# Attention ahead of two mixture-of-experts layers: block averages of the values with the values as the stationary operand

## Chip, cores and metric

The kernel runs on one core of one Trainium2 chip. The metric is the device time of one launch in microseconds. The kernel before took 1074.11 us, the median of three timed runs (1064.62, 1074.11 and 1075.32 us).

## What is computed

Inputs are q, k and v of shape (4, 8, 768, 64), 4 batch elements with 8 heads, float32, and the weights of two expert layers. The change is in the attention alone:

```python
block, window = (32, 16)
nb = S // block                                   # 24 blocks of 32 keys
k_sum = k.reshape(B, H, nb, block, D).max(axis=3)
v_sum = v.reshape(B, H, nb, block, D).mean(axis=3)
scores_l = scale * np.matmul(q, k.transpose(0, 1, 3, 2))       # masked to |i - j| < 16
scores_s = scale * np.einsum('bhsd,bhnd->bhsn', q, k_sum) + np.log(block)
a = softmax(np.concatenate([masked scores_l, scores_s], axis=-1))
out = np.matmul(a, np.concatenate([v, v_sum], axis=2))
```

Each query attends to the keys nearer than 16 and to 24 block summaries: the maximum of each block's keys, the mean of each block's values. Its output, 3072 tokens of 512, goes through a layer of 8 experts (each token to its best expert, hidden size 1024) and a second such layer in which each expert takes 384 tokens.

## The kernel before

One program, with an instruction stream written out by hand for each of five engines (TensorE, VectorE, ScalarE, GpSimd, called POOL in the profile, and SyncE, called SP), tied by semaphores. The stages follow each other: attention, routing of the first layer, its experts, routing of the second layer and its experts interleaved.

**Work of the attention.** The heads are taken in pairs (hp, four pairs for each of four batch elements, 16 pairs in all). A pair has 12 query blocks of 64 (j); a block sees a span of 96 keys (`WK`) and the 24 block summaries, 120 rows (`PW`) in all. The values come from the host cut into these spans, `va[hp]`: 96 rows of keys, then 24 rows in which the block means are put. For each query block and head they hold 64 values and a column of ones, which gives the softmax's denominator in the same matmul.

A pair is three units (n = 3 hp, 3 hp + 1, 3 hp + 2) of four query blocks. The units are software-pipelined with one order on every engine, in the functions `unit` of each block. In unit n TensorE issues: `scores(n)` (L670), `transpose_probs(n-2)` (L679), then, if n % 3 is 1, `means` of the next pair m (L689), then `values(n-3)` (L707), `transpose_rows(n-4)` (L721) and, for each batch element's last pair, the router's `first_logits(n-5)` (L730). VectorE: `maxima(n)` (L1231, L1234), `take_means` (L1204) if n % 3 is 1, `normalise(n-3)` (L1240, L1242, L1247), and `block_maxima` (L1186) of the next pair's keys. ScalarE does the exponentials and the copies out of PSUM. POOL works by pairs: `key_spans(m)` (L518, L519, L521) cuts the keys into spans, `spread_means(m)` (L528) spreads the means over the 12 blocks of `va`. The loop over the first three batch elements is a hardware loop; the first 6 units stand before it and the last element's behind it.

**The means before.** `average` is a table of 96 x 12 x 24 numbers made on POOL (L534, four times L532): 1/32 where a span's key row belongs to a block. For each of the 12 spans a matmul has the 24 columns of `average[:, j, :]` stationary (weights) and 128 columns of values (two heads) moving, and all 12 add up in 24 rows (96 to 119) of a PSUM bank, `MEAN0` onwards, in the bank that `values(n-3)` of the same unit writes. `take_means` copies them to `vst`, waiting for that unit's values (`pv_done`), and `spread_means` copies `vst` into `va`. `values` of the pair wait for that (`vsum_done`).

In float32 each such matmul is two passes on TensorE: the profile counts two MATMUL (PE) and two LDWEIGHTS (PEld) for one; its transposes are one pass.

Of the kernel before, what the change touches and what calls it, by code (L numbers as in the profile page):

```python
# [10 lines left out]
ALU = mybir.AluOpType  # L11
# [4 lines left out]
P = 128  # L16
B, H, S, D = 4, 8, 768, 64
BLOCK, WINDOW = 32, 16
NB = S // BLOCK
# [20 lines left out]
MEAN0 = 2 * GU * VD  # L40
MASKED = -1e30
# [71 lines left out]
def two_layers_of_experts(nc, queries, k, v_win, modality_id, w_gate, modality_bias, w1, w2,  # L113
                          w_gate2, w1b, w2b, out):
    ctx = ExitStack()
    with ctx:
# [133 lines left out]
        means_made = sem("means_made")  # L250
        means_taken = sem("means_taken")
# [38 lines left out]
        average = sa("average", [WK, NQ, NB])  # L290
# [4 lines left out]
        va = [sa(f"va{i}", [PW, 2, NQ, VD]) for i in range(HP)]  # L295
# [106 lines left out]
        def _(sp):  # L402
# [4 lines left out]
            def load_v(b, hp):  # L407
                sp.dma_start(va[hp][0:WK, :, :, :], v_win[bass.ds(b, 1), hp, :, :, :, :].rearrange("o p h j w -> (o p) h j w")
                             ).then_inc(vw_loaded[hp], 16)
# [78 lines left out]
        def _(pool):  # L488
# [35 lines left out]
            def spread_means(m):  # L524
                pool.wait_ge(means_taken, m + 1)
                if m >= HP:
                    pool.wait_ge(pv_done, PU * (m - HP + 1))
                chain(g.tensor_copy(va[m % HP][WK:PW, :, :, 0:D], vst[m % 2][WK:PW, :, :].unsqueeze(2).to_broadcast([NB, 2, NQ, D])))  # L528
                g.nop().then_inc(vsum_done, 1)

            avg = average[:, :, :]
            pick = lambda pattern, base, per: chain(g.affine_select(out=avg, in_=avg, compare_op=ALU.is_ge, fill=0.0, base=base,  # L532
                                                                    pattern=pattern, channel_multiplier=per))
            chain(g.memset(avg, 1.0 / BLOCK))  # L534
            pick([[QB, NQ], [-BLOCK, NB]], -WINDOW, 1)
            pick([[-QB, NQ], [BLOCK, NB]], WINDOW + BLOCK - 1, -1)
            pick([[-2, NQ], [1, NB]], 0, 0)
            pick([[2, NQ], [-1, NB]], 1, 0)
            for t in va:
                chain(g.memset(t[WK:PW, :, :, D:VD], 1.0))  # L540
# [113 lines left out]
        def _(pe):  # L654
# [38 lines left out]
            def values(b, n):  # L693

                hp, i = n // PU, n % PU
                if i == 0:
                    pe.wait_ge(vsum_done, HP * b + hp + 1)
                pe.wait_ge(pt_out, UNITS * b + n + 1)
                if n >= 2:
                    pe.wait_ge(x_done, UNITS * b + n - 1)  # L700
                else:
                    pe.wait_ge(means_taken, 2)
                for t in range(GU):
                    for h in range(2):
                        a = 2 * t + h
                        for s_ in range(2):
                            last = mm(bank[4 + n % 2][QB * s_:QB * s_ + QB, VD * a:VD * a + VD], pt[n % 2][:, a, QB * s_:QB * s_ + QB],  # L707
                                      va[hp % HP][:, h, 2 * (GU * i + t) + s_, :], start=True, stop=True)
                last.then_inc(pv_done, 1)
# [27 lines left out]
            def unit(b, n, own):  # L737
# [4 lines left out]
                if n == 0:  # L742
                    pe.wait_ge(const_ready, 1)
                    means(0, 0, 0)
                if n % PU == 1:
                    m = n // PU + 1
                    own(means, PU * m, m, n)
# [418 lines left out]
        def _(dve):  # L1166
# [30 lines left out]

            def take_means(b, m, n):
# [37 lines left out]
            def normalise(b, m):  # L1236
                hp, i = m // PU, m % PU
                ps = bank[4 + m % 2][:, 0:2 * GU * VD].rearrange("p (a w) -> p a w", w=VD)
                dve.wait_ge(pv_done, UNITS * b + m + 1)
                vec.tensor_scalar(rtmp[:, :], ps[:, :, D], 1e-9, None, ALU.add).then_inc(sums_read, 1)  # L1240
# [3 lines left out]
                if i == 0:  # L1244
# [3 lines left out]
                                  ps[:, :, 0:D].rearrange("p (t h) d -> p t h d", h=2),  # L1248
                                  rinv[:, :].rearrange("p (t h) -> p t h", h=2).unsqueeze(3).to_broadcast([P, GU, 2, D]), ALU.mult).then_inc(x_done, 1)

            def unit(b, n, own):

                own(maxima, n, n)
                m = n // PU + 1
                if n == 0:
                    take_means(0, 0, 0)
                if n % PU == 1:
                    own(take_means, PU * m, m, n)
# [460 lines left out]
def laid_out(inputs):  # L1719
# [9 lines left out]
    rows = _np.ones((B, HP, WK, 2, NQ, VD), v.dtype)  # L1729
    rows[..., :D] = _np.where(outside[:, :, None], 0, v[:, :, :, key, :]).transpose(0, 1, 4, 2, 3, 5)  # L1730
# [26 lines left out]
```

## Time and profile before

| | |
|---|---|
| median of three timed runs | 1074.11 us |
| lowest and highest | 1064.62, 1075.32 us |
| the profiled execution's own time | 1066.68 us |
| its span, first to last instruction | 1064.9 us |
| TensorE busy | 898.2 us, 84% |
| VectorE busy | 681.6 us, 64% |
| mean granted TensorE clock | 0.925 of 2.4 GHz |

The profile is of one execution. PE is TensorE's matmuls, PEld its weight loads, which run beside them; DVE is VectorE, ACT ScalarE. An "L" number is a line of the kernel. "Idle before" is time in which the engine stood still ahead of an instruction, with what ended it. The granted clock is 1.00 at 2.4 GHz and 0.50 at 1.2 GHz. Two levels are all that occur. Times within the span are counted from its first instruction.

### The profile page before, as it was taken

The numbers are of one execution on the slowest core, as the hardware profiler recorded it, in microseconds if no ns is written. First come the engines' busy times: TensorE is split into PE (matmuls) and PEld (weight loads), VectorE is DVE, ScalarE is ACT, GpSimd is POOL, SyncE is SP. The second block draws the span as 40 slices with busy tenths as digits, with TensorE's granted clock in tenths as the row PEclk, the third lists the DMA queues.
The fourth block names the chain that finished last, engine by engine and source line by source line (L and its number), as shares of the span: only waits on it lengthen the run. The fifth ranks groups of instructions, "written<-read, shape, count | busy, mean of one in ns | idle before, by whom it ended". The sixth has DMA issues, their size and how long they took to land.

```text
span 1064.9 us, 21948 instructions
## 1 busy us (share of the span) xinstructions
PE 898.2 (84%) x7342; PEld 733.7 (69%) x7343; DVE 681.6 (64%) x1998; ACT 305.5 (29%) x626; POOL 285.1 (27%) x390
## 2 busy tenths in 40 slices
PE   4899999915899999999996233999898989998995
PEld 3787878714688888888885122868686867687884
DVE  5757576575666666666665567777777768674440
ACT  2544454505322212222221003223232322223330
POOL 5733344101012111111220005050515151414501
PEclk9999999956899999999998655999999999999998
DMA  9676675915011111111110123414141414155100
GB/s 195 122 160 135 133 153 100 280 50 185 11 51 40 50 40 40 40 40 40 40 50 20 24 71 119 159 51 169 50 169 54 165 61 159 61 204 172 32 29 30
DMA packets 45631, 99.94 MB, mean 94 GB/s; under 512 B 6736, under 2 KB 19072, under 8 KB 45440
## 3 DMA queue, kind: packets, MB, share of 16 engines
q1 hardware_dynamic: 26816, 61.63, 19.8%
q0 software_dynamic: 8064, 26.46, 7.9%
q10 hardware_dynamic: 10688, 11.01, 4.9%
q8 instruction: 39, 0.64, 0.2%
q14 instruction: 24, 0.20, 0.1%
HBM read 79.57 MB, written 19.51 MB: 93 GB/s over the span
## 4 chain that ended last, share of the span: by engine, by line
PE 69%; DVE 18%; issue 4%; POOL 3%; ACT 2%; DMA 2%; DVEq 0%; ACTq 0%; SPq 0%; POOLq 0%
PE bank L777 27%; PE bank L898 11%; PE bank L912 9%; PE bank L689 4%; PE bank L670 3%; PE bank L848 3%; DVE w_low L1649 2%; PE bank L730 2%; PE bank L707 2%; PE bank L801 2%; PE bank L679 2%; POOL slot_hot L635 2%; DVE xl L1653 1%; DVE ge L1517 1%; ACT xh L1042 1%
## 5 line engine op out<-in xcount | busy, mean ns | idle before, releaser
L1404 DVE SCALAR_TENSOR_TENSOR bank<-y,wg 128x512 f32<-128x512 f32 x200 | 132.0, 723 | 2.9
L635 POOL TENSOR_SCALAR slot_hot<-iota_l,mlo 128x128 bf16<-128x128 f32 x96 | 72.0, 766 | 214.7 <-DVE mlo L1622 214.7
L898 PE MATMUL bank<-xh,w_high 128*128 128x384 f32 x256 | 94.3, 368 | 16.1 <-DVE hl L1639 8.9
L777 PE MATMUL bank<-w_high,hh 128*128 x200 | 83.2, 416 | 13.2 <-DVE hl L1393 13.2
L777 PE MATMUL bank<-w_high,xh 128*128 x200 | 82.7, 414 | 10.7 <-DVE gates L1386 10.7
L592 POOL DMA_INDIRECT y_rows<-y,sidx x25 | 25.0, 998 | 243.2 <-DVE bank L1404 243.2
L898 PE MATMUL bank<-xh,w_low 128*128 128x384 f32 x256 | 88.1, 344 | 0.0
L898 PE MATMUL bank<-xl,w_high 128*128 128x384 f32 x256 | 87.9, 344 | 0.0
L1042 ACT ACTIVATE hh<-bank 128x512 fp32r<-128x512 f32 x50 | 27.1, 595 | 203.1 <-PE bank L801 203.1
L1418 DVE TENSOR_SCALAR y<-bank,gates 128x512 f32<-128x512 f32 x25 | 18.8, 751 | 101.1 <-PE bank L777 101.1
L912 PE MATMUL bank<-w_high,hh 128*128 128x512 f32 x192 | 82.3, 429 | 0.0
L1042 ACT ACTIVATE w_high<-w_landed 128x1024 fp32r<-128x1024 f32 x64 | 63.1, 1049 | 66.0 <-DMA w_landed<-in_moe_w 66.0
L777 PE MATMUL bank<-w_low,hh 128*128 x200 | 80.5, 403 | 0.0
L777 PE MATMUL bank<-w_high,hl 128*128 x200 | 80.3, 402 | 0.0
L777 PE MATMUL bank<-w_low,xh 128*128 x200 | 80.3, 402 | 0.0
L777 PE MATMUL bank<-w_high,xl 128*128 x200 | 80.2, 401 | 0.0
L1649 DVE TENSOR_TENSOR w_low<-w_landed,w_high 128x1024 fp32r<-128x1024 f32 x64 | 77.8, 1219 | 0.8
L848 PE MATMUL bank<-ge,cb 128*8 128x16 bf16 x1344 | 42.3, 170 | 41.7 <-DVE ge L1517 41.6
L912 PE MATMUL bank<-w_high,hl 128*128 128x512 f32 x192 | 75.7, 394 | 0.0
L912 PE MATMUL bank<-w_low,hh 128*128 128x512 f32 x192 | 75.5, 393 | 0.0
L848 PEld LDWEIGHTS bank<-ge,cb 128*8 128x8 bf16 x1344 | 36.2, 83 | 54.6 <-DVE ge L1517 50.8
L1118 ACT ACTIVATE hh<-bank 128x384 fp32r<-128x384 f32 x64 | 31.5, 492 | 140.2 <-PE bank L898 140.2
(285 smaller groups left out, 1932.5 us busy)
## 6 DMA issues: line engine op xcount, KB each, us to landing
w_landed<-in_moe_w SPq DMA_DIRECT2D x16, 2048.0 KB, 10.5
va<-in_v_win SPq DMA_DIRECT2D x16, 585.0 KB, 6.4
raw_w<-in_moe_w SPq DMA_DIRECT2D x4, 2048.0 KB, 11.3
k_raw<-in_k SPq DMA_DIRECT2D x16, 384.0 KB, 9.1
q_eye<-in_q ACTq DMA_DIRECT2D x16, 384.0 KB, 7.4
x_rows<-x ACTq DMA_DIRECT2D x12, 384.0 KB, 10.2
wg<-in_moe_w_gate SPq DMA_DIRECT2D x1, 2048.0 KB, 25.8
x_rows<-x SPq DMA_DIRECT2D x4, 387.0 KB, 7.2
```

The source lines that it names most:

```text
L592: pool.indirect_dma_start(out=dst[:, :], out_offset=bass.IndirectOffsetOnAxis(ap=sidx[:, 0:1], axis=0), in_=y[:, 0:w], in_offset=None).the ...
L635: last = g.tensor_scalar(slot_hot[:, j, :], iota_l[:, :], mlo[:, j:j + 1], None, ALU.is_equal)
L670: last = mm(bank[n % 2][QB * s_:QB * s_ + QB, PW * (2 * t + h):PW * (2 * t + h) + PW], qe[hp % 2][:, h, QB * j:QB * j + QB], kbt[hp % 2][: ...
L689: last = mm(bank[4 + (n + 1) % 2][WK:PW, MEAN0:MEAN0 + 2 * D], average[:, j, :], va[m % HP][0:WK, :, j, 0:D], start=j == 0, stop=j == NQ - 1)
L777: last = mm(ps, lhs[a][:, c, :], rhs[b](c), start=c == 0 and t == 0, stop=c == n - 1 and t == 2)
L848: last = mm(bank[7][0:E, 0:KSEARCH], cb[:, j, :], ge[:, j, :], start=j == 0, stop=j == TC - 1)
L898: last = mm(bank[fc % 2][:, 0:CAP], w[:, q % 2, c, f], a[:, c, :], start=c == 0 and t == 0, stop=c == KC - 1 and t == 2)
L912: last = mm(bank[2 + t % 2][:, :], a[:, c, rows], w[:, q % 2, c, :], start=c == 0 and n == 0, stop=c == FC - 1 and n == 2)
L1042: copy = lambda o, a: nc.scalar.activation(o, a, ACT.Copy)
L1118: nc.scalar.activation(hh2[:, fc, :], bank[fc % 2][:, 0:CAP], ACT.Relu).then_inc(hhigh_done, 1)
L1404: stt(bank[6 + e % 2][:, :], y[:, 0:DM], 1.0, wg2[:, e, :], ALU.mult, ALU.mult, accum_out=y[:, DM + e:DM + e + 1]).then_inc(l2_out, 1)
L1649: tt(low, whole, high.bitcast(F32), ALU.subtract).then_inc(low_done, 1)
```

## The change

The averaging matmul is turned round. The values of one span, 128 columns (both heads), are now the stationary operand, and `average` is 96 x 2: a span starts 16 keys ahead of its 64 queries, and rows 16 to 47 and 48 to 79 are its two blocks. Each of the 12 matmuls (`block_sums`) gives two columns of 128 (the block means of both heads, head dimension down the partitions); together they fill 24 columns of a bank, 128 x 24. VectorE copies them to `v_sums` (`take_sums`), and one unit later a single matmul against the identity (`means`, stationary `v_sums`, two passes) turns them into the 24 x 128 that there was before. So that the stationary operand is one row of 128 in memory, `va` is laid out anew: for each span a column of ones, 64 values of head 0, 64 of head 1, a column of ones. `normalise` reads its denominators and values at their new places. The host lays out `v_win` to match, with the same number of bytes.

```diff
-        average = sa("average", [WK, NQ, NB])
+        average = sa("average", [WK, 2])
+        vsums = [sa(f"v_sums{i}", [P, NB]) for i in range(2)]
...
-        va = [sa(f"va{i}", [PW, 2, NQ, VD]) for i in range(HP)]
+        va = [sa(f"va{i}", [PW, NQ, 2 * VD]) for i in range(HP)]
...
-                chain(g.tensor_copy(va[m % HP][WK:PW, :, :, 0:D], vst[m % 2][WK:PW, :, :].unsqueeze(2).to_broadcast([NB, 2, NQ, D])))
+                chain(g.tensor_copy(va[m % HP][WK:PW, :, 1:1 + 2 * D], vst[m % 2][WK:PW, :, :].rearrange("p h d -> p (h d)").unsqueeze(1).to_broadcast([NB, NQ, 2 * D])))
...
             chain(g.memset(avg, 1.0 / BLOCK))
-            pick([[QB, NQ], [-BLOCK, NB]], -WINDOW, 1)
-            pick([[-QB, NQ], [BLOCK, NB]], WINDOW + BLOCK - 1, -1)
-            pick([[-2, NQ], [1, NB]], 0, 0)
-            pick([[2, NQ], [-1, NB]], 1, 0)
+            chain(g.affine_select(out=avg, in_=avg, compare_op=ALU.is_ge, fill=0.0, base=-WINDOW, pattern=[[-BLOCK, 2]], channel_multiplier=1))
+            chain(g.affine_select(out=avg, in_=avg, compare_op=ALU.is_ge, fill=0.0, base=WINDOW + BLOCK - 1, pattern=[[BLOCK, 2]], channel_multiplier=-1))
             for t in va:
-                chain(g.memset(t[WK:PW, :, :, D:VD], 1.0))
+                chain(g.memset(t[WK:PW, :, 0:1], 1.0))
+                chain(g.memset(t[WK:PW, :, 2 * VD - 1:2 * VD], 1.0))
...
+            def block_sums(b, m, n):
+                pe.wait_ge(vw_loaded[m % HP], 16 * (b + m // HP + 1))
+                if m or not isinstance(b, int):
+                    pe.wait_ge(sums_taken, HP * b + m)
+                if n >= 5:
+                    pe.wait_ge(x_done, UNITS * b + n - 4)
+                for j in range(NQ):
+                    last = mm(bank[4 + (n + 1) % 2][:, SUM0 + 2 * j:SUM0 + 2 * j + 2], va[m % HP][0:WK, j, 1:1 + 2 * D], average[:, :], start=True, stop=True)
+                last.then_inc(sums_made, 1)
+
             def means(b, m, n):
-                pe.wait_ge(vw_loaded[m % HP], 16 * (b + m // HP + 1))
+                pe.wait_ge(sums_taken, HP * b + m + 1)
...
-                for j in range(NQ):
-                    last = mm(bank[4 + (n + 1) % 2][WK:PW, MEAN0:MEAN0 + 2 * D], average[:, j, :], va[m % HP][0:WK, :, j, 0:D],
-                              start=j == 0, stop=j == NQ - 1)
-                last.then_inc(means_made, 1)
+                mm(bank[4 + (n + 1) % 2][WK:PW, MEAN0:MEAN0 + 2 * D], vsums[m % 2][:, :], ident[:, :], start=True, stop=True).then_inc(means_made, 1)
...
+            def take_sums(b, m, n):
+                dve.wait_ge(sums_made, HP * b + m + 1)
+                if n >= 3:
+                    dve.wait_ge(pv_done, UNITS * b + n - 2)
+                if m >= 2:
+                    dve.wait_ge(means_made, HP * b + m - 1)
+                vec.tensor_copy(vsums[m % 2][:, :], bank[4 + (n + 1) % 2][:, SUM0:SUM0 + NB]).then_inc(sums_taken, 1)
```

In `unit`, on TensorE and on VectorE alike, the new functions stand where `means` and `take_means` stood (n % 3 is 1), and `means` and `take_means` move to the next unit (n % 3 is 2); in unit 0 both stand one behind the other.

TensorE's stream, two units of the loop (n % 3 is 1 and 2), before; L689 is the averaging, L707 the values, L721 the transposed rows:

```order
L670 MATMUL bank<-k_bias,q_eye 64x120 x8
L679 MATMUL bank<-ident,probs 120x128 x4
L683 ISA
L689 MATMUL bank<-va,average 24x128 x12
L707 MATMUL bank<-va,pt 64x65 x8
L721 MATMUL bank<-ident,x 128x128 x2
L665 REGISTER_ALU
L670 MATMUL bank<-k_bias,q_eye 64x120 x8
L679 MATMUL bank<-ident,probs 120x128 x4
L707 MATMUL bank<-va,pt 64x65 x8
```

And the same place of the changed kernel (L671, L680, L715 and L729 are the former L670, L679, L707 and L721; L690 is `block_sums`, L699 the turn):

```order
L671 MATMUL bank<-k_bias,q_eye 64x120 x8
L680 MATMUL bank<-ident,probs 120x128 x4
L684 ISA
L690 MATMUL bank<-average,va 128x2 x12
L715 MATMUL bank<-va,pt 64x65 x8
L729 MATMUL bank<-ident,x 128x128 x2
L666 REGISTER_ALU
L671 MATMUL bank<-k_bias,q_eye 64x120 x8
L680 MATMUL bank<-ident,probs 120x128 x4
L694 REGISTER_ALU
L699 MATMUL bank<-ident,v_sums 24x128
L715 MATMUL bank<-va,pt 64x65 x8
```

The twelve matmuls stay where they are with another shape, and one more stands in the unit behind them, between the transposed probabilities and the values.

VectorE's stream at the same two units, before (L1204 is the copy of the means, L1240 to L1247 normalise, L1186 the block maxima):

```order
L1231 TENSOR_REDUCE nmax<-bank 128x4
L1234 TENSOR_SCALAR nmax<-nmax 128x4
L1199 REGISTER_ALU
L1203 REGISTER_ALU
L1204 COPY vst<-bank 24x128
L1240 TENSOR_SCALAR rtmp<-bank 128x4
L1242 RECIPROCAL rinv<-rtmp 128x4
L1247 TENSOR_TENSOR x<-bank,rinv 128x2x128
L1186 TENSOR_REDUCE ksum<-k_raw 64x24
```

And in the changed kernel, where L1251 to L1268 are the former L1231 to L1247, L1216 is the new copy and L1224 the copy of the means:

```order
L1251 TENSOR_REDUCE nmax<-bank 128x4
L1254 TENSOR_SCALAR nmax<-nmax 128x4
L1211 REGISTER_ALU
L1215 REGISTER_ALU
L1216 COPY v_sums<-bank 128x24
L1261 TENSOR_SCALAR rtmp<-bank 128x4
...
L1198 TENSOR_REDUCE ksum<-k_raw 64x24
...
L1254 TENSOR_SCALAR nmax<-nmax 128x4
L1224 COPY vst<-bank 24x128
L1261 TENSOR_SCALAR rtmp<-bank 128x4
```

The new copy takes the place of the old one ahead of normalise and the block maxima; the old one stands ahead of the next unit's normalise.

## Rows read from the trace of the kernel before

**Rows 1.** The page: granted TensorE clock in 40 equal slices, in tenths.

```profile
PEclk9999999956899999999998655999999999999998
```

**Rows 2.** Stretches: length; busy PE, PEld, DVE, ACT, POOL; granted clock; DMA share, GB/s.

```profile
20.00:40.00 20.00, 17.40 (x232) 14.12 (x228) 14.40 (x29) 7.56 (x23) 12.48 (x24) 1.00 0.58 135
...
120.00:140.00 20.00, 20.00 (x235) 17.32 (x235) 12.40 (x32) 9.02 (x29) 8.93 (x12) 0.91 0.46 101
...
180.00:200.00 20.00, 18.90 (x260) 15.30 (x261) 16.77 (x45) 11.89 (x38) 6.89 (x8) 1.00 0.56 151
```

**Rows 3.** TensorE's waits, 20 to 205 us: total us, times, longest.

```profile
PE bank L670 <- POOLq L522: 4.2, 7, 1.3
PE bank L721 <- DVE x L1247: 1.9, 3, 1.3
```

**Rows 4.** Groups of instructions, TensorE, 20 to 200 us: busy us, mean ns.

```profile
L730 PE MATMUL bank<-wg,xt 128*128 128x8 f32 x144 | 16.7, 251 | 0.0
...
L730 PEld LDWEIGHTS bank<-wg,xt 128*128 128x128 f32 x144 | 16.8, 192 | 0.0
```

**Rows 5.** Timeline of TensorE, 140 to 151 us: start, us.

```profile
141.04 2.80 PE L689 MATMUL bank<-va,average 96*24 96x128 f32 x24
143.78 0.69 PE L707 MATMUL bank<-va,pt 120*64 120x65 f32 x16
144.39 0.44 PE L721 MATMUL bank<-ident,x 128*128 128x128 f32 x2
144.76 1.04 PE L670 MATMUL bank<-k_bias,q_eye 128*64 128x120 f32 x16
145.73 0.65 PE L679 MATMUL bank<-ident,probs 128*120 128x128 f32 x4
146.31 0.69 PE L707 MATMUL bank<-va,pt 120*64 120x65 f32 x16
```

**Rows 6.** Timeline of TensorE, 66 to 82 us.

```profile
74.27 1.85 PE L730 MATMUL bank<-wg,xt 128*128 128x8 f32 x16
76.05 1.04 PE L670 MATMUL bank<-k_bias,q_eye 128*64 128x120 f32 x16
```

**Rows 7.** Groups by shape, 0 to 250 us: copies of the means, and their nearest.

```profile
L1240 DVE TENSOR_SCALAR rtmp<-bank 128x4 f32<-128x4 f32 x48 | 7.5, 156 | 3.4 <-PE bank L707 3.0
...
L1204 DVE COPY vst<-bank 24x128 f32<-24x128 f32 x16 | 4.7, 297 | 36.0 <-PE bank L707 29.6 <-PE bank L689 6.3
```

**Rows 8.** POOL's wait, 20 to 240 us.

```profile
POOL k_bias L521 <- DVE ksum L1186: 91.8, 14, 8.5
```

**Rows 9.** Timelines of TensorE and POOL at the start.

```profile
14.35 5.32 PE L689 MATMUL bank<-va,average 96*24 96x128 f32 x24 [0.24 <-POOLq L541]
...
20.91 2.80 PE L689 MATMUL bank<-va,average 96*24 96x128 f32 x24
...
9.18 2.60 POOL L532 TENSOR_SCALAR_AFFINE_SELECT average<-average 96x288 f32<-96x288 f32 x4
```

**Rows 10.** The drop at 133 us: timeline of TensorE, then busy time and clock.

```profile
131.08 1.85 PE L730 MATMUL bank<-wg,xt 128*128 128x8 f32 x16
132.86 1.81 PE L670 MATMUL bank<-k_bias,q_eye 128*64 128x120 f32 x16
134.60 1.11 PE L679 MATMUL bank<-ident,probs 128*120 128x128 f32 x4
135.64 1.01 PE L707 MATMUL bank<-va,pt 120*64 120x65 f32 x16
136.58 0.44 PE L721 MATMUL bank<-ident,x 128*128 128x128 f32 x2
...
133.00:136.40 3.40, 3.40 (x34) 2.76 (x34) 2.99 (x5) 0.75 (x2) 2.83 (x3) 0.50 0.00 0
```

**Rows 11.** The last L730 group: busy time (PE, PEld) and clock.

```profile
211.50:214.80 3.30, 3.28 (x16) 3.19 (x15) 0.50 0.96 369
209.80:211.40 1.60, 1.60 (x17) 1.60 (x16) 1.00 1.00 401
```

More of the change, by code:

```diff
@@ L40 @@
 MEAN0 = 2 * GU * VD
+SUM0 = MEAN0 + 2 * D
 MASKED = -1e30
@@ L250, in two_layers_of_experts @@
         means_made = sem("means_made")
+        sums_made = sem("sums_made")
+        sums_taken = sem("sums_taken")
         means_taken = sem("means_taken")
@@ L407, in load_v @@
             def load_v(b, hp):
-                sp.dma_start(va[hp][0:WK, :, :, :], v_win[bass.ds(b, 1), hp, :, :, :, :].rearrange("o p h j w -> (o p) h j w")
+                sp.dma_start(va[hp][0:WK, :, :], v_win[bass.ds(b, 1), hp, :, :, :].rearrange("o p j w -> (o p) j w")
                              ).then_inc(vw_loaded[hp], 16)
@@ L527, in spread_means @@
                     pool.wait_ge(pv_done, PU * (m - HP + 1))
-                chain(g.tensor_copy(va[m % HP][WK:PW, :, :, 0:D], vst[m % 2][WK:PW, :, :].unsqueeze(2).to_broadcast([NB, 2, NQ, D])))
+                chain(g.tensor_copy(va[m % HP][WK:PW, :, 1:1 + 2 * D], vst[m % 2][WK:PW, :, :].rearrange("p h d -> p (h d)").unsqueeze(1).to_broadcast([NB, NQ, 2 * D])))
                 g.nop().then_inc(vsum_done, 1)
-            avg = average[:, :, :]
-            pick = lambda pattern, base, per: chain(g.affine_select(out=avg, in_=avg, compare_op=ALU.is_ge, fill=0.0, base=base,
-                                                                    pattern=pattern, channel_multiplier=per))
+            avg = average[:, :]
             chain(g.memset(avg, 1.0 / BLOCK))
-            pick([[QB, NQ], [-BLOCK, NB]], -WINDOW, 1)
-            pick([[-QB, NQ], [BLOCK, NB]], WINDOW + BLOCK - 1, -1)
-            pick([[-2, NQ], [1, NB]], 0, 0)
-            pick([[2, NQ], [-1, NB]], 1, 0)
+            chain(g.affine_select(out=avg, in_=avg, compare_op=ALU.is_ge, fill=0.0, base=-WINDOW, pattern=[[-BLOCK, 2]], channel_multiplier=1))
+            chain(g.affine_select(out=avg, in_=avg, compare_op=ALU.is_ge, fill=0.0, base=WINDOW + BLOCK - 1, pattern=[[BLOCK, 2]], channel_multiplier=-1))
             for t in va:
-                chain(g.memset(t[WK:PW, :, :, D:VD], 1.0))
+                chain(g.memset(t[WK:PW, :, 0:1], 1.0))
+                chain(g.memset(t[WK:PW, :, 2 * VD - 1:2 * VD], 1.0))
             g.nop().then_inc(const_ready, 1)
@@ L707, in values @@
                             last = mm(bank[4 + n % 2][QB * s_:QB * s_ + QB, VD * a:VD * a + VD], pt[n % 2][:, a, QB * s_:QB * s_ + QB],
-                                      va[hp % HP][:, h, 2 * (GU * i + t) + s_, :], start=True, stop=True)
+                                      va[hp % HP][:, 2 * (GU * i + t) + s_, VD * h:VD * h + VD], start=True, stop=True)
                 last.then_inc(pv_done, 1)
@@ L743, in unit @@
                     pe.wait_ge(const_ready, 1)
+                    block_sums(0, 0, 0)
                     means(0, 0, 0)
                 if n % PU == 1:
+                    m = n // PU + 1
+                    own(block_sums, PU * m, m, n)
+                if n % PU == 2:
                     m = n // PU + 1
@@ L1237, in normalise @@
                 hp, i = m // PU, m % PU
-                ps = bank[4 + m % 2][:, 0:2 * GU * VD].rearrange("p (a w) -> p a w", w=VD)
+                ps = bank[4 + m % 2][:, 0:2 * GU * VD].rearrange("p (t w) -> p t w", w=2 * VD)
+                rows2 = lambda a: a[:, :].rearrange("p (t h) -> p t h", h=2)
                 dve.wait_ge(pv_done, UNITS * b + m + 1)
-                vec.tensor_scalar(rtmp[:, :], ps[:, :, D], 1e-9, None, ALU.add).then_inc(sums_read, 1)
+                vec.tensor_scalar(rows2(rtmp), ps[:, :, 0:2 * VD:2 * VD - 1], 1e-9, None, ALU.add).then_inc(sums_read, 1)
                 dve.wait_ge(sums_read, UNITS * b + m + 1)
@@ L1247, in normalise @@
                 vec.tensor_tensor(x[:, GU * i:GU * i + GU, c:c + P].rearrange("p t (h d) -> p t h d", h=2),
-                                  ps[:, :, 0:D].rearrange("p (t h) d -> p t h d", h=2),
+                                  ps[:, :, 1:1 + 2 * D].rearrange("p t (h d) -> p t h d", h=2),
                                   rinv[:, :].rearrange("p (t h) -> p t h", h=2).unsqueeze(3).to_broadcast([P, GU, 2, D]), ALU.mult).then_inc(x_done, 1)
@@ L1255, in unit @@
                 if n == 0:
+                    take_sums(0, 0, 0)
                     take_means(0, 0, 0)
                 if n % PU == 1:
+                    own(take_sums, PU * m, m, n)
+                if n % PU == 2:
                     own(take_means, PU * m, m, n)
@@ L1728, in laid_out @@
     laid["k"] = k.transpose(0, 1, 4, 2, 3)
-    rows = _np.ones((B, HP, WK, 2, NQ, VD), v.dtype)
-    rows[..., :D] = _np.where(outside[:, :, None], 0, v[:, :, :, key, :]).transpose(0, 1, 4, 2, 3, 5)
+    rows = _np.ones((B, HP, WK, NQ, 2 * VD), v.dtype)
+    for h in range(2):
+        rows[..., 1 + D * h:1 + D * h + D] = _np.where(outside[:, :, None], 0, v[:, :, h, key, :]).transpose(0, 1, 3, 2, 4)
     laid["v_win"] = rows
```

## The prediction

> **What bounds the kernel now.** I read the page first: TensorE is busy for 84% of the span, and its granted clock [rows 1] is 9 tenths or more in the slices that hold the attention stage, the only one that the change touches. The busy time by stretches of 20 us [rows 2] then says how tight that stage is: from 20 us on TensorE is busy for 17.40, 20.00 and 18.90 of 20.00 us, VectorE for 14.40, 12.40 and 16.77. So in this stage time on TensorE is time on the clock. The list of TensorE's waits [rows 3] is short: over 185 us it lost 4.2 us to the copy of the keys' spans (POOL) and 1.9 us to VectorE's x, the two longest entries. Everything put on TensorE shows, apart from what falls into those few microseconds.
>
> A pair's old means are 12 matmuls of two passes, 24 passes. The timeline [rows 5] gives their price by differences of starts: the group starts at 141.04 and the next at 143.78, so 2.74 us, 0.114 us a pass. All groups below are measured so, from start to start.
>
> **Part 1, the matmuls turned round.** Twelve matmuls remain twelve, so still 24 passes a pair, but now each loads 128 columns of weights and streams 2, where the old one loads 24 and streams 128. The operation in the trace that is built like this is the router's product L730: 128 columns loaded, 8 streamed. It starts at 74.27 and its follower at 76.05 [rows 6]: 1.78 us for 16 passes, 0.111 us each. Streaming 16 times fewer columns has bought nothing there: weight loads fill its time (over nine such groups PEld is busy for 16.8 us, PE for 16.7 [rows 4]). For the block sums: 24 x 0.111 = 2.67 us against 2.74, a gain of 0.07 us a pair, about 1 us in all. Bounds: below, the cheapest pass of the stage, L707's (143.78 to 144.39, 16 passes, 0.038 us each [rows 5]), would make 0.92 us, 1.8 us less a pair; above, each weight load alone, nothing beside it, 0.192 us [rows 4], would make 4.6 us, 1.9 us more. I take L730's, the row of the same shape. The skill's rule (the Trainium skill, "TensorE: Matmul & The Clock Gate", on LDWEIGHTS) is that a weight load takes its column count over 1.2 ns and that the number of rows does not matter; that makes 107 ns a pass and 2.56 us a group, and would close the one gap in the likeness, 96 rows here and 128 in L730, whose 111 ns a pass agree with it.
>
> **Part 2, the turn.** One matmul of two passes a pair, a unit later, between L680 and L715. Two passes at 0.114 are 0.23 us; as dear as the whole group of four L679 transposes it would be 0.58 (145.73 to 146.31 [rows 5]), and two of those, the nearest row, are 0.29. I take 0.3: 15 in the stage make 4.5 us. It stands in the unit ahead of the scores that begin a pair, and that is where TensorE waits for POOL's spans (4.2 us, 7 times, at most 1.3 [rows 3]); some of those waits cover it. I book 3 us; without cover 4.5, and 8.7 at the upper bound.
>
> **Part 3, VectorE.** Sixteen more copies, out of PSUM, 128x24. The nearest rows are 128x4 at 0.156 us and 24x128 at 0.297 [rows 7]: 2.5 to 4.8 us on an engine that has 3.2 us or more free in each 20 of those rows [rows 2]. In the unit with the sums the new copy takes the place of the longer one, so what stands behind it (normalise, then the block maxima for which POOL and the next pair's scores wait) is not later; in the next unit the old copy stands ahead of normalise, which TensorE needs a unit later. I book 0; with the cover gone it would be up to 4.8 us.
>
> **Part 4, POOL.** The spread copy keeps its size (24 partitions, 1536 elements each), and begins when the copy of the next unit is done. Behind it in POOL's queue stand the span copies of the next pair, and behind those a wait for the maxima that lasted 91.8 us in 14 times, 6.6 us each [rows 8]. A shift of a microsecond or two vanishes there. The normalise reads and the value matmuls keep their sizes. 0.
>
> **Part 5, the start.** The first means wait 0.24 us for POOL's constants [rows 9]; POOL builds a 2-column table in place of one of 288, of which four selections alone took 2.60 us, so that wait goes: -0.24. But in unit 0 the turn now follows its sums at once: TensorE must wait for VectorE's copy and pay two slow passes (5.32 / 24 x 2 = 0.44 us), with the copy (0.30) and the handovers (0.1) some 0.8 us. Net +0.6.
>
> **Part 6, the clock.** Here the sum is decided. The attention stage has one drop [rows 10]: the granted clock is 1.00 up to 133, 0.50 from 133.0 to 136.4, 1.00 after. What TensorE did just before it fell is a group of L730. It fell again at 211.5, in the middle of L730's last group: from 209.8 to 211.4 TensorE was busy 1.60 of 1.60 us at 1.00, and from 211.5 to 214.8 for 3.28 of 3.30 us at 0.50 [rows 11]. None of the other 14 groups of old means in the stage has a drop behind it (at 20 to 40 and 180 to 200 us the clock stands at 1.00, and only 120 to 140, with the drop described, has less [rows 2]). So the engine was not idle, it was loading weights with little streamed behind each load. The block sums are this pattern, purer (2 columns for 8) and longer (2.7 us in one piece for 1.8), once a pair, 15 times in some 180 us. The skill has a rule against this: in the same page, "What's actually happening", the clock goes to 1.2 GHz after an idle stretch. By that rule TensorE, which would be busy all through, keeps 2.4 GHz and this part is nothing (rival A). The row at 211.5 says otherwise.
>
> The price of one drop is in rows 10: the L670, L679 and L707 groups after it took 1.74, 1.04 and 0.94 us (132.86, 134.60, 135.64, 136.58), against 0.97, 0.58 and 0.61 at full clock (from 144.76, 145.73 and 143.78 on [rows 5]): 3.72 - 2.16 = 1.56 us. I expect one behind each block-sum group from the third on: 14 x 1.56 = 21.8 us. At the start the clock is still low (the first group takes 5.32 us) and the second, at 20.91, already runs at full clock in 2.80 us [rows 9]. Behind a first group that streams next to nothing I expect it still slow: at L730's pace at 0.50 (16 passes in 3.3 us, 0.206 each [rows 11]) it takes 4.9 us, +2.1, and the scores beside it about +0.9 more: +3.
>
> **Sum.** The profiled execution took 1066.68 us (its span and 1.8 us around it). 1066.7 - 1 + 3 + 0 + 0 + 0.6 + 21.8 + 3 = 1094.1. The median of the three timed runs, 1074.11, is 7.4 us higher; I go about half way and predict 1097 us.
>
> **The rivals.**
> A, the clock holds. Place: behind the block sums. For it: nine groups of L730 run in this stage (144 passes of 16 [rows 4]) and only one is followed by a drop. Against it: those are shorter, stream four times as much and stand among other matmuls. It decides if the granted clock stays at 1.00 in the stage. Then 1066.7 - 1 + 3 + 0.6 = 1069.3, or 1076.7 on the median: not slower by what can be told.
> B, the passes are cheap. If the 96-row loads are hidden as L707's are, the group falls to 0.92 us: 16 x 1.82 = 29 us off, 1066.7 - 29 + 3.6 = 1041. Against it stands L730, whose 16 passes take 1.78 us whatever is streamed. It decides from a pass below 0.085 us (11 us in all).
> C, the sums themselves fall into the slow stretches. A group at 0.50 costs 24 x (0.206 - 0.111) = 2.3 us more; if each of 15 did so, 15 x (1.56 + 2.3) = 58 us, and 1066.7 + 2.6 + 58 = 1127. For it: a slow group streams no more than a fast one, so nothing in it brings the clock back. Against it: at 136.4 the clock came back after the groups that also follow the block sums.
>
> **How the numbers follow.** Forecast 0.66, A 0.22, B 0.04, C 0.08. A measurement of this kernel tells about 1% (11 us) from no change. Slower by over 1%: the forecast and C, 0.74. Within 1%: A, 0.22. Faster: B, 0.04. The range runs from the middle of A, 1072 (some of the groups pull the clock down, or none), to 1112, the forecast with the uncovered costs of parts 2 and 3 (+1.5 and +4.8) and four slow groups of C (+9). Left out are B, most of C and about half of A.
>
> **What would show it.** Right: block sums at 2.6 to 2.8 us from start to start with weight loads filling them; TensorE's granted clock at 0.50 for 10 to 17 short stretches between 20 and 230 us, each beginning in or just behind block sums; the attention stage ending 20 to 35 us later; everything after it unchanged. Wrong: a clock of 1.00 through the stage (A); passes of the block sums well under 0.1 us (B); turns that wait for VectorE beyond the first; the rest of the program changing its length.

## The result and the profile after

The changed kernel takes 1097.82 us (median of four runs, 1091.85 to 1102.25) against 1071.99 us of the kernel before (four runs, one more than in the table above), a ratio of 1.0256 with a 95% interval of 1.0202 to 1.0311: 2.6% slower, 26 us. The profiled execution took 1094.77 us, its span 1093.0.

First the page, at the line that answers to [rows 1], the granted clock in slices of 27 us:

```profile
PEclk9977888885799999999999755799999999999998
```

Before, the first eight slices read 9 and the next two 5 and 6; now the third to the ninth read 7 and 8. These slices lie in the attention stage. The first slice reads 9 in both kernels although its first matmuls ran at the slow pace (below): the clock's record begins with the first rise, at 20.3 us before and 32.3 after, and what lies ahead of it counts as full. So the clock is better read from the first rise on. Here it is in one row, up to just ahead of the stage's end, for the changed kernel:

```profile
33.00:236.00 203.00, 202.06 (x2268) 170.71 (x2264) 115.04 (x326) 92.89 (x287) 72.09 (x108) 0.84 0.61 135
```

and for the kernel before (length, then busy PE, PEld, DVE, ACT, POOL, then the granted clock):

```profile
21.00:209.00 188.00, 179.51 (x2310) 147.74 (x2310) 125.03 (x320) 96.12 (x295) 76.31 (x112) 0.99 0.70 151
```

TensorE is busy for 202 of 203 us, at a mean clock of 0.84; VectorE, with one small copy a pair more, is less busy per us (115 of 203 us, for 125 of 188). The trace's clock record gives what the mean is made of: from 33 us to the end of the attention the clock is at 0.50 in 13 stretches, 64.8 us together, against one stretch of 3.4 us before. Four of them, by their rows, and ahead of them the row of the 5.2 us before the first fall:

```profile
44.09:49.30 5.21, 5.21 (x65) 4.80 (x66) 2.71 (x10) 1.99 (x6) 3.44 (x17) 1.00 1.02 196
49.30:52.70 3.40, 3.40 (x26) 2.36 (x28) 2.74 (x6) 1.98 (x6) 2.73 (x5) 0.50 1.06 103
59.60:66.40 6.80, 6.80 (x56) 5.29 (x56) 2.53 (x7) 1.98 (x6) 0.66 (x1) 0.50 0.57 117
73.20:80.00 6.80, 6.80 (x58) 5.29 (x59) 2.53 (x7) 1.98 (x6) 0.66 (x1) 0.50 0.54 91
90.30:100.50 10.20, 10.20 (x77) 8.88 (x77) 3.17 (x11) 2.17 (x7) 0.66 (x1) 0.50 0.01 2
```

TensorE was not idle ahead of the fall: it was busy for 5.21 of 5.21 us at 1.00. All 13 falls come within 4.2 us of the start of a block-sum group: eight inside the group and five 1.1 to 1.6 us behind its end. Each of the 13 groups from 45 us on has one, which is what the prediction had set as its sign.

What stands where the old means stood [rows 5] is in TensorE's timeline of the changed kernel (start, us):

```profile
45.55 2.74 PE L690 MATMUL bank<-average,va 96*128 96x2 f32 x24
48.22 0.69 PE L715 MATMUL bank<-va,pt 120*64 120x65 f32 x16
48.83 0.44 PE L729 MATMUL bank<-ident,x 128*128 128x128 f32 x2
49.20 1.80 PE L671 MATMUL bank<-k_bias,q_eye 128*64 128x120 f32 x16
50.93 1.11 PE L680 MATMUL bank<-ident,probs 128*120 128x128 f32 x4
51.97 0.62 PE L699 MATMUL bank<-ident,v_sums 128*24 128x128 f32 x2
52.52 0.77 PE L715 MATMUL bank<-va,pt 120*64 120x65 f32 x16
53.22 0.44 PE L729 MATMUL bank<-ident,x 128*128 128x128 f32 x2
```

The block sums take 48.22 - 45.55 = 2.67 us. At 49.3, 1.1 us later, the clock falls, and the scores behind them take 1.73 us in place of 0.97, the transposed probabilities 1.04 for 0.58, the turn 0.55 for 0.33, the values 0.70 for 0.61: 1.53 us lost, until 52.7. The fall at 59.6 comes inside the next block sums (they start at 57.59), and the slow stretch lasts 6.8 us.

TensorE's waits from 20 to 230 us, once 4.2 and 1.9 us [rows 3], have shrunk to one row:

```profile
PE bank L729 <- DVE x L1268: 0.5, 1, 0.5
```

TensorE, now slower, hardly waits for anyone. The start has changed too; there the first two groups of old means took 5.32 and 2.80 us [rows 9], and now it reads:

```profile
13.41 5.25 PE L690 MATMUL bank<-average,va 96*128 96x2 f32 x24 [0.84 <-DMA va<-in_v_win]
18.93 0.62 PE L699 MATMUL bank<-ident,v_sums 128*24 128x128 f32 x2 [0.27 <-DVE v_sums L1216]
19.48 1.87 PE L671 MATMUL bank<-k_bias,q_eye 128*64 128x120 f32 x16
21.28 5.28 PE L690 MATMUL bank<-average,va 96*128 96x2 f32 x24
```

Both groups now run at the low clock, which rises at 32.3 us and not at 20.3.

**Where the 28 us of span come from.** The scores of the seventh unit start at 37.1 us before and 41.0 after: 3.9 us at the start. The last product of the attention ends at 214.8 before and 242.1 after: 27.3 us, so 23.4 in what is called the steady stage below, from the seventh scores to the end of the attention (177.7 us before, 201.1 after). All that follows, the experts' stages with it, is 0.8 us longer together.

### The profile page after: what moved, and what is told of

The parts are those of the page before. It is cut to its first block, busy times and chain, and to the rows that moved or that the text cites. A ratio compares the mean times of both kernels' runs of the same rounds, so it can differ in the third digit from the quotient of the medians.

```text
span 1093.0 us, 22071 instructions
## 1 busy us (share of the span) xinstructions
PE 934.7 (86%) x7374; PEld 767.9 (70%) x7375; DVE 674.4 (62%) x2014; ACT 305.3 (28%) x626; POOL 283.6 (26%) x392
## 4 chain that ended last, share of the span: by engine, by line
PE 73%; DVE 15%; issue 3%; ACT 2%; DMA 2%; POOL 2%; DVEq 0%; SPq 0%; ACTq 0%; POOLq 0%
PE bank L789 25%; PE bank L910 11%; PE bank L924 9%; PE bank L671 5%; PE bank L690 4%; PE bank L715 3%; PE bank L680 3%; PE bank L860 3%; PE bank L738 2%; DVE w_low L1673 2%; PE bank L813 2%; PE bank L729 2%; POOL slot_hot L636 2%; DVE xl L1677 1%; DVE ge L1541 1%
## 5 line engine op out<-in xcount | busy, mean ns | idle before, releaser
L789 PE MATMUL bank<-w_high,hh 128*128 x200 | 83.0, 415 | 13.8 <-DVE hl L1417 13.5
L593 POOL DMA_INDIRECT y_rows<-y,sidx x25 | 24.9, 998 | 245.7 <-DVE bank L1428 245.7
L671 PE MATMUL bank<-k_bias,q_eye 128*64 128x120 f32 x768 | 62.5, 317 | 10.7 <-DVE k_bias L1208 10.7
```

What stands on the lines that cost most here:

```text
L671: last = mm(bank[n % 2][QB * s_:QB * s_ + QB, PW * (2 * t + h):PW * (2 * t + h) + PW], qe[hp % 2][:, h, QB * j:QB * j + QB], kbt[hp % 2][: ...
L789: last = mm(ps, lhs[a][:, c, :], rhs[b](c), start=c == 0 and t == 0, stop=c == n - 1 and t == 2)
```

## The experiments

Each is compared with runs of the kernel before on the same chip. "Stretches" are those at half clock between the first rise and the end of the attention, without the one in which it ends.

**e1: 100 columns streamed.** Is it the thin streaming, or the turn with its copies and waits?

```diff
-        average = sa("average", [WK, 2])
+        average = sa("average", [WK, 100])
...
-                    last = mm(bank[4 + (n + 1) % 2][:, SUM0 + 2 * j:SUM0 + 2 * j + 2], va[m % HP][0:WK, j, 1:1 + 2 * D], average[:, :], start=True, stop=True)
+                    last = mm(bank[4 + (n + 1) % 2][:, SUM0 + 2 * j:SUM0 + 2 * j + 100], va[m % HP][0:WK, j, 1:1 + 2 * D], average[:, :], start=True, stop=True)
```

> The changed kernel, but the averaging table has 100 columns instead of 2 (the other 98 are 1/32), so each block-sum matmul streams 100 columns behind the same load of 128; the 98 extra results land where the next matmul or nobody reads. Theory (the clock): weight loads already take 0.111 us a pass and 100 streamed columns take less, so the group keeps its 2.67 us, the drops behind block sums disappear, the attention's granted clock is 1.00 but for one or two stretches, and the time is that of before plus the turn, 1070 to 1080 us against 1098. Rival (the turn, the copies and their waits cost the time): 1095 to 1100 us as before the edit. Rival (the 128-column weight loads pull the clock down, whatever is streamed): drops and time stay, 1095 to 1100 us.

Measured: 1068.97 us against 1069.23, ratio 1.0002 (0.9975 to 1.0029, 12 runs). No stretch at half clock between the first rise and the one in which the attention ends. Timeline, then the stage in one row:

```profile
104.80 2.82 PE L690 MATMUL bank<-average,va 96*128 96x100 f32 x24
107.55 0.69 PE L715 MATMUL bank<-va,pt 120*64 120x65 f32 x16
```

```profile
33.00:210.00 177.00, 174.66 (x2258) 148.06 (x2254) 114.79 (x327) 93.01 (x287) 72.35 (x109) 1.00 0.74 149
```

The group lasts 0.08 us longer (2.75 us), TensorE streams fifty times the columns in it, and the loss against the kernel before is gone. Turn, copies, layout, 128-column loads and all waits are still in. Both rivals fall. Against the changed kernel the steady stage takes 174.6 us for 201.1: these 26.5 us are what streaming 2 columns in place of 100 costs, and the slow stretches go with them.

That e1 is level with the kernel before is in part a balance. Its seventh scores start at 41.0 us, as late as in the changed kernel, so the 3.9 us of the start are still lost. Its steady stage is 3.1 us shorter than the 177.7 us of before: it has no drop like the one at 133 us, and TensorE is idle in it for 2.3 us in place of 6.9.

**e2: 8 columns, and e7: 32 columns.** The same edit with 8 and with 32 for 100.

> The same with 8 columns streamed, the shape of the router's L730. Theory: still next to nothing is streamed in 2.7 us, so the drops stay, 12 to 18 of them, and the time is 1090 to 1102 us. Rival (only the turn costs): the same time, but then e1 has it too.

> The changed kernel with 32 columns streamed in place of 2 (8 gave 1097.5 us and 11 stretches at half clock, 100 gave 1069 and none). Theory: in between, fewer drops than with 8, 2 to 9, 1072 to 1090 us. Rival (only all or nothing counts): 11 to 13 drops and 1095 us.

Measured: 1097.54 us with 8 (one run, 11 stretches, 58.0 us at half clock) and 1079.45 us with 32 (one run, 8 stretches, 34.1 us). The stage's rows, 8 columns and then 32:

```profile
33.00:235.00 202.00, 199.40 (x2259) 168.40 (x2256) 113.85 (x324) 92.68 (x286) 71.97 (x108) 0.86 0.65 136
```

```profile
33.00:224.00 191.00, 189.18 (x2252) 160.45 (x2252) 114.30 (x324) 92.80 (x285) 72.33 (x108) 0.91 0.67 147
```

With 2, 8, 32 and 100 columns the clock's mean is 0.84, 0.86, 0.91 and 1.00 and the time 1098, 1098, 1079 and 1069 us, while the weights loaded and the passes are the same in all four. The two in the middle are single runs, and 2 and 8 columns are not told apart in time.

**e3: the turn alone.** Added to the kernel before, in the unit behind its means:

```diff
+            def extra_turn(b, m, n):
+                if n >= 5:
+                    pe.wait_ge(x_done, UNITS * b + n - 4)
+                mm(bank[4 + (n + 1) % 2][WK:PW, MEAN0 + 2 * D:MEAN0 + 4 * D - 4], ident[:, 0:NB], ident[:, 0:2 * D - 4], start=True, stop=True)
```

> The kernel before with one more matmul a pair where the changed kernel has its turn (24 columns loaded, 124 streamed, 15 times; its result is not used), without the copy on VectorE. Theory: no drops, TensorE gets 15 x 0.33 = 5 us more, some of it hidden in the waits for POOL: plus 2 to 5 us, 1074 to 1077 us. Rival (the turn, with its change of shape, is what costs 26 us): 1090 us or more.

Measured: 1069.31 us against 1069.23, ratio 0.9989 (0.9967 to 1.0012, 12 runs). The upper end allows 1.3 us, less than expected. In the profiled execution:

```profile
107.23 0.39 PE L696 MATMUL bank<-ident 128*24 128x124 f32 x2
107.56 0.69 PE L712 MATMUL bank<-va,pt 120*64 120x65 f32 x16
```

It takes its 0.33 us (107.56 - 107.23), 5 us in the stage, but over the 12 runs next to nothing of it reaches the time. Why is not shown. In the profiled execution (1071.07 us) TensorE is idle for 5.5 us of the steady stage in place of 6.9, so the waits there took in 1.4 us and not 4 or 5. That execution also has an early start: the clock rises at 15.9 us (20.3 before) and the seventh scores start at 35.2 (37.1), though TensorE's first matmuls are the same. So a start differs by about 2 us from one execution to another.

**e5, e6 and e9: thin streaming behind light loads.** The kernel before, with its 24-column loads, streaming 2 columns (one matmul of a group 128), done three and four times, so that a thin stretch is as long as the changed kernel's. e5 is the same done once. All three leave out most of the averaging; they are for the time alone.

```diff
-                for j in range(NQ):
-                    last = mm(bank[4 + (n + 1) % 2][WK:PW, MEAN0:MEAN0 + 2 * D], average[:, j, :], va[m % HP][0:WK, :, j, 0:D],
-                              start=j == 0, stop=j == NQ - 1)
+                for j in range(3 * NQ):
+                    last = mm(bank[4 + (n + 1) % 2][WK:PW, MEAN0:MEAN0 + (2 if j else 2 * D)], average[:, j % NQ, :],
+                              va[m % HP][0:WK, 0:(1 if j else 2), j % NQ, 0:(2 if j else D)], start=True, stop=True)
```

> The kernel before, but 11 of the 12 averaging matmuls of a pair stream 2 columns in place of 128 (24 columns loaded as before); the means are then not the block means. It tells what a nearly free averaging would be worth and whether thin streaming in a short group does anything to the clock. Theory: the group lasts 0.9 to 1.2 us, too short to bring the clock down in most places, 0 to 5 drops, 1045 to 1058 us.

> The same with the twelve done three times, 36 matmuls of 24 loaded and 2 streamed columns (one streams 128), so that the thin stretch is 2.3 to 3 us long again; again the means are not the block means. Theory (little streamed brings the clock down): drops behind these groups as in the changed kernel, 8 to 16 of them, 1085 to 1100 us. Rival (loads of 128 columns do it): at most 3 drops, 1063 to 1075 us.

> e6 with the twelve done four times: 96 passes of 24 loaded and 2 streamed columns at 0.0286 us each, 2.75 us, the length of the changed kernel's group (e6's lasted 2.06 us and had 5 stretches at half clock, 27 us in all, within the stage). The means are again not the block means. Theory (the length of a thin stretch decides, not what is loaded): 9 to 14 stretches, 45 to 70 us at half clock before the end of the stage, which comes at 235 to 245 us; 1085 to 1100 us. Rival (loads of 128 columns do most of it): as e6, 5 or 6 stretches, and only the 11 us that the longer groups take on top of it, 1074 to 1078 us.

Measured, one run each. e5: 1054.87 us, 5 stretches, 17.1 us at half clock, a group of 0.86 us. e6: 1065.35 us, 5 stretches, 27.3 us, a group of 2.06 us. e9: 1140.94 us, 14 stretches, 129.7 us. The groups in the timelines of e5, e6 and e9, in this order (a merged row shows the shape of its first matmul, here 128 columns):

```profile
150.70 0.93 PE L689 MATMUL bank<-va,average 96*24 96x128 f32 x24
151.56 0.63 PE L707 MATMUL bank<-va,pt 120*64 120x65 f32 x14
```

```profile
145.53 2.13 PE L689 MATMUL bank<-va,average 96*24 96x128 f32 x72
147.59 0.69 PE L707 MATMUL bank<-va,pt 120*64 120x65 f32 x16
```

```profile
72.60 2.73 PE L689 MATMUL bank<-va,average 96*24 96x128 f32 x96
75.27 0.69 PE L707 MATMUL bank<-va,pt 120*64 120x65 f32 x16
```

e5 came out as expected. e6 missed the theory's 1085 us and 8 stretches; its time lies in the rival's range (1063 to 1075 us) and its 5 stretches in neither. Its group is a quarter shorter than the changed kernel's. e9, at the full 2.67 us, overshot the theory by 40: there the clock is low for longer than in any other kernel, but TensorE was also short of instructions, in waits on "issue" that its weight loads show (these lines of the kernel before have 27.8 us in their stage, none over 1.6):

```profile
PEld bank L670 <- issue: 18.1, 35, 4.6
PEld bank L679 <- issue: 17.5, 35, 5.7
PEld bank L707 <- issue: 12.5, 33, 4.6
```

So e9's time is not the clock's alone and is no measure of it. e5 has a like flaw: TensorE is idle for 14.0 us of its steady stage, before for 6.9. e6 is the cleanest, with 7.9 us idle, and has 27 us at half clock where the kernel before has 3.4. So loads of 128 columns are not needed: 24-column loads with thin streaming bring the clock down too. From e5 to e9 the half-clock time grows with the length of the group (17, 27, 130 us), one run each and e9's with the idle time in it.

**e12: the same sums in three runs.** The twelve are split in fours: ahead of the unit's scores, behind them, and behind the transposed probabilities.

```diff
+                m = n // PU + 1
+                if n % PU == 1:
+                    own(block_sums, PU * m, m, n, range(0, 4))
                 own(scores, n, n)
+                if n % PU == 1:
+                    own(block_sums, PU * m, m, n, range(4, 8))
...
-                    own(block_sums, PU * m, m, n)
+                    own(block_sums, PU * m, m, n, range(8, NQ))
```

> The changed kernel with the twelve block sums of a pair in three runs of four in the same unit: ahead of the scores, behind them, and behind the transposed probabilities. Same matmuls, same 24 passes, same 2 columns; only the thin stretch of 2.67 us becomes three of 0.9 us in 4.2 us, with dense work between them. Theory (the length of the thin stretch decides): fewer stretches at half clock than 13 before the end of the attention, 3 to 9, and 1075 to 1090 us. Rival (the sum of thin passes decides, however they stand): 12 to 14 stretches and 1095 to 1100 us.

Measured: 1099.32 us, ratio 1.0293 (1.0245 to 1.0341, 4 runs); 8 stretches, but longer ones, 68.3 us together. The stage:

```profile
33.00:237.00 204.00, 202.96 (x2270) 173.98 (x2269) 115.38 (x327) 93.07 (x286) 72.27 (x109) 0.83 0.61 129
```

The theory as I put it here fell. That the thin stretch is broken up by dense work twice gains nothing; over a unit the amount of thin work is the same, and the time at half clock about the same. The rival's words ("the sum of thin passes") fit, though not its count of stretches.

**e10 and e11: the start.** 28 transposes of the identity ahead of the first scores, in the changed kernel (e10) and in e1 (e11).

```diff
+            pe.wait_ge(eye_ready, 1)
+            for _ in range(28):
+                tr(bank[7][:, 0:P], ident[:, :], ident[:, :])
             pe.wait_ge(bias_rows, 1)
```

> The changed kernel with the 28 transposes of e8 ahead of the first scores. In the changed kernel and in e1, e2 and e7 the clock first rose at 29.5 to 32.3 us, in the others at 15.9 to 26.4. Theory: the late rise costs 3 to 4 us and is apart from the drops behind the block sums; with the clock up at the first scores the first block sums run in 2.7 us and the seventh scores start at 36 to 38 us instead of 41.0, the drops stay, 1091 to 1096 us. Rival (the first two block-sum groups bring the clock down at once, warm or not): scores at 40 to 42 us, 1095 to 1100 us.

> e1 (100 columns streamed) with the 28 transposes ahead of the first scores, as e10 has them on the changed kernel. In e10 the clock was up at 8.0 us, fell at 14.9 in the first block sums and was back at 31.9. Theory: streaming 100 columns, the block sums don't pull it down; the clock stays at 1.00 from about 8 us on, the seventh scores start at 32 to 35 us instead of e1's 41.1, and the time is 1060 to 1066 us against e1's 1069. Rival (something else than the columns streamed holds the start down): the clock is at 0.50 until about 31 us again and the seventh scores start at 39 to 41 us.

Measured: e10 1091.07 us, ratio 1.0202 (1.0143 to 1.0261, 4 runs), not told apart from the changed kernel's 1.0256; 13 stretches after the start, 58.0 us. e11 1073.11 us, ratio 1.0000 (0.9965 to 1.0036, 10 runs), no gain over e1. In both the clock rises early and falls again. e10, then e11:

```profile
8.00:13.60 5.60, 2.67 (x31) 2.26 (x30) 5.28 (x11) 0.00 (x0) 4.81 (x13) 1.00 1.06 220
15.00:31.80 16.80, 16.52 (x99) 14.04 (x99) 6.06 (x12) 3.23 (x11) 5.30 (x6) 0.50 0.82 163
```

```profile
9.00:15.60 6.60, 4.26 (x45) 3.86 (x44) 4.86 (x10) 1.11 (x4) 5.74 (x13) 1.00 1.15 217
15.80:29.30 13.50, 13.23 (x81) 11.06 (x82) 5.22 (x10) 2.64 (x9) 3.09 (x4) 0.50 0.81 170
```

The seventh scores start at 40.3 us (e10) and 38.9 (e11), against 41.0 in both without the transposes and 37.1 in the kernel before. So at the start both rivals were right, to within 1.6 us (e10's time, 1091 us, is what the theory gave). Thin streaming is not needed for the late start: e1 and e11 stream 100 columns and have it. Ahead of the fall TensorE had been busy for only 2.67 of 5.60 us in e10 and 4.26 of 6.60 us in e11, so the transposes did not test a start without idle time. After the fall it was busy for 13.23 of 13.50 us in e11 and the clock still stayed at 0.50.

**e4 and e8: the old orientation in four column groups.** The twelve matmuls of the kernel before are dealt to four column groups of the array; the four partial sums are copied by VectorE and added by one matmul in the place of the turn. e8 adds the transposes of e10 and moves one POOL load behind the constants.

```diff
-                    last = mm(bank[4 + (n + 1) % 2][WK:PW, MEAN0:MEAN0 + 2 * D], average[:, j, :], va[m % HP][0:WK, :, j, 0:D],
-                              start=j == 0, stop=j == NQ - 1)
+                    last = mm(bank[4 + (n + 1) % 2][32 * (j % 4):32 * (j % 4) + 32, MEAN0:MEAN0 + 2 * D], average[:, j, :], va[m % HP][0:WK, :, j, 0:D],
+                              start=j < 4, stop=j >= NQ - 4)
...
+                mm(bank[4 + (n + 1) % 2][WK:PW, MEAN0:MEAN0 + 2 * D], fold[:, :], vsums[m % 2][:, :], start=True, stop=True).then_inc(means_made, 1)
```

> The old orientation, but the 12 averaging matmuls of a pair go to four column groups of the array in turn (32 columns loaded, outputs at partitions 0, 32, 64, 96, three matmuls adding up in each); VectorE copies the four parts (128x128) and one matmul with a stacked identity adds them, a unit later, where the changed kernel has its turn. Theory: passes on different column groups run beside each other as L670's two do, 0.04 us a pass or less, the group takes 0.7 to 1.0 us instead of 2.74, the turn gives back 0.3: 16 x 1.5 = 24 us saved, 1045 to 1055 us, with at most a few drops of the clock. Rival (the groups don't overlap at four): the group stays at 2.7 us and the time is 1075 to 1080 us. Rival (the stage is then bound by VectorE and POOL): group short, but TensorE waits 10 us more and the time is 1058 to 1068 us.

> The four column groups of e4, with two changes at the start: TensorE does 28 transposes of the identity into an unused bank while it would wait for the first keys, and POOL issues its load of the modalities behind the constants instead of ahead of them. Theory: the clock is at 1.00 when the first scores start, or a few us later, the first means no longer wait 2.3 us for POOL: 4 to 8 us less than e4, 1052 to 1057 us. Rival (what is saved at the start is waited for later, at the keys of the next pairs): 1058 to 1061 us.

Measured: e4 1059.86 us, ratio 0.9909 (0.9872 to 0.9945, 6 runs), e8 1055.73 us, ratio 0.9868 (0.9839 to 0.9896, 6 runs). Both are faster than the kernel before by 1%, clear of their intervals; e8 is not told apart from e4. e4's group, and TensorE's waits in the attention:

```profile
105.94 0.87 PE L696 MATMUL bank<-va,average 96*32 96x128 f32 x24
106.74 0.69 PE L722 MATMUL bank<-va,pt 120*64 120x65 f32 x16
```

```profile
PE bank L677 <- POOLq L526: 5.6, 3, 3.1
...
PE bank L677 <- DMA q_eye<-in_q: 3.3, 2, 2.1
PE bank L736 <- DVE x L1274: 2.7, 3, 1.1
```

24 passes in 0.80 us in place of 2.74: four groups run beside each other. That is 1.9 us less a pair, 31 us in all, of which 9 to 10 reach the time. The time is that of e4's second rival. In the profiled execution the attention ends 15.8 us earlier (199.0 for 214.8): the added turns take some 5 us, the waits for keys' spans, queries and VectorE's x some 5 more than before (TensorE is idle for 11.9 us of the steady stage, for 6.9), and one more stretch at half clock 1.5. Another 3.9 us are lost behind the attention (854.0 us from its end to the program's, for 850.2); why was not followed. e5 says the same from another side: with the averaging nearly free (0.86 us a pair) the gain was 15 us, in one run.

## Why the prediction was right

The forecast was 1097 us and the measurement 1097.82, in the direction and by the mechanism named. That the number fits to a microsecond is luck: the spread of the four runs is 10 us, and several parts below were off and cancelled. By its parts:

- **Part 1 (24 passes of L730's kind, 2.67 us a pair, -1 us)**: measured 2.67 us. The rule of the Trainium skill ("TensorE: Matmul & The Clock Gate", "LDWEIGHTS") gave an estimate of 2.56 and the row 2.67. Rival B is out: 96 rows load no faster than 128 in this shape.
- **Part 2 (turn, 0.3 us each, +3)**: each takes 0.33 us at full clock, but the booked 3 us look too many: e3's runs leave it 1.3 us at the most. The cover is not the reason that the trace shows, since e3's waits took in only 1.4 us; what took in the rest stays open.
- **Part 3 and part 4 (VectorE's copies, POOL's spread, 0)**: the new copy takes 0.183 us (16 of them 2.9), between my two rows. e1, which has both, is level with the kernel before, and its TensorE waits less. Right.
- **Part 5 (the first turn, +0.6)**: the turn waits 0.27 us for the copy. The first means no longer wait for POOL, but for their own values (0.84 us, a DMA), which I did not name; they still start 0.94 us earlier, since the first scores did (10.70 for 12.24). This too I had missed. The five copies of VectorE that the first scores wait for took 2.23 us in place of 3.48; in the kernel before, POOL ran its four selections of 288 columns beside them. What the rest of part 5 came to is within the 3.9 us of the start.
- **Part 6, the drops (14 x 1.56 = 21.8)**: 13 stretches. One of 3.4 us costs 1.53 us (the timeline above). But five of the 13 are longer, so that 64.8 us at half clock stand against my 14 x 3.4 = 48. At 1.53 us for 3.4 us that is 29, less the 1.5 us of the one drop before that is gone; against it stand the 6 us that TensorE no longer waits (0.9 us idle in the steady stage for 6.9). With the 13 turns that fall into this stage, 4.3 us, and part 1's 0.9 it gives 29 - 1.5 - 6 + 4.3 - 0.9 = 24.9, where 23.4 were measured. The sum came out because two misses cancel: longer stretches than forecast, and waits that the slow engine no longer has. Rival C's own price hardly came: the 13 groups lost 1.6 us together by running in part at half clock.
- **Part 6, the start (+3)**: the size came out (3.9 with part 5, I had 3.6), but from two misses: counted from the first scores to the seventh, the start is 5.4 us longer (30.3 for 24.9), and the first scores are 1.5 us earlier. The cause I named is not borne out. I put it down to the first group's thin streaming; e1 has the late rise of the clock (31.2 us) and the same start (41.0) with 100 columns streamed, and e11 a late one even after an early rise. The step "behind a first group that streams next to nothing I expect it still slow" is true of what happened, but thin streaming is not needed for it.

Rival A fell with the result. The Trainium skill's sentence on the idle stretch ("TensorE: Matmul & The Clock Gate", "What's actually happening") does not cover this case: TensorE was busy for 5.21 of 5.21 us ahead of the fall at 49.3, and for 6.80 of 6.80 us at 0.50 from 59.6 on. That the time comes back when the same passes stream more is shown by e1; that the rows at 133 and 211 us of the kernel before told as much was an inference then.

Open: what holds the clock down at the start of the kernels with 128-column block sums. It was up (but for the short drops) at 29.4 to 33.0 us in all seven of them, and at 15.9 to 30.2 in the other seven kernels, one execution each; of the spread, 4.4 us are between two with the same start (before and e3). Open too is how the amount of thin work and its distribution combine: e12 excludes only that a single unbroken stretch decides. And the runs vary the columns streamed; what it is in thin streaming that brings the clock down they do not tell.

## What to carry to other kernels

A matmul that loads many weight columns and streams very few costs twice (128 loaded and 2, 8 or 32 streamed here): its passes are no shorter, and a run of them, though TensorE is 100% busy, can halve the clock of the dense work behind it. Before turning operands round, look for a group of the same shape in the trace and at the granted clock just behind it; if the stage is bound by TensorE, count the time at half clock (here 0.45 us lost for each us of it), not the columns saved. Where many small matmuls use few output columns, dealing them to the array's column groups is worth more (24 passes in 0.80 us for 2.74), up to the point at which another engine's waits take over.

## What was not expected of the hardware

- Padding a matmul with useless columns made the kernel 27 us faster (e1's span of 1065.6 us against the changed kernel's 1093.0), at no cost in the group's length beyond 0.08 us.
- Breaking thin work up with dense work between did not help (e12): fewer stretches, 8 for 13, and as much time at half clock, 68.3 us for 64.8 in the changed kernel.
- 28 transposes ahead of the first scores brought the clock up at 8.0 to 10.4 us, but it fell again at 13.8 to 15.7 in all three kernels that have them (e8, e10, e11).
- With 96 averaging passes a pair in place of 24 (e9), TensorE's matmuls stood still on "issue" for 26 us of the stage, up to 5.3 us at a time, where the kernel before has 1.1 us; e6, with 72, has 3.4.
